# Attention and two mixture stages on one core: first loads on two queues, products with v one batch later, v loaded a pair later

## The chip, the cores and the metric

The kernel runs on one core of one Trainium2 chip. The metric is the device time of one execution in microseconds (us), the median of three runs.

## The reference

Three stages follow one another: windowed attention with sink tokens, a dense layer pair with a softmax-gated unit and a layer norm, and a sum over eight experts. The change touches the first stage alone.

```
batch, n_heads, seq, head_dim = (2, 8, 768, 64);  n_sink, window = (4, 128)
scores = scale * np.matmul(q, k.transpose(0, 1, 3, 2))
keep = (pos[None, :] < n_sink) | ((rel >= 0) & (rel < window))     # rel = query - key
scores = np.where(keep, scores, -1000000000.0)
a = np.exp(scores - np.max(scores, axis=-1, keepdims=True))
a = a / (np.sum(a, axis=-1, keepdims=True) + 1e-09)
x = np.matmul(a, v)                              # (2, 8, 768, 64), then 1536 tokens x 512
h = x @ w_in;  solu = h * softmax(h);  x = layernorm(solu) * g_ln @ w_out
out = sum over e of P[:, e:e+1] * (np.maximum(x @ w1[e], 0.0) @ w2[e])   # P: 8 Sinkhorn rounds
```

## The kernel before

**Tiling.** The 16 heads of attention are worked as 8 pairs (p = 0 to 7); the two heads h of a pair lie on partitions 0 to 63 and 64 to 127 of `q_sb` and `k_sb`. Each head has six query tiles of 128 rows (t = 0 to 5). A tile needs its own 128 keys, the 128 before them and the four sink keys: 128, 256 and then 260 columns. The buffers `q_sb`, `k_sb`, `v_sb`, `v_sink` and `probs` exist twice, one for even and one for odd pairs.

**What happens to a pair.** Every engine runs a program of its own, in which the work is written out in the order in which it is to run; semaphores tie the programs together.

- TensorE: `scores(p, t)` (line 643) makes the scores of a tile for both heads into four banks in turn. `turn(p, b)` (line 663) transposes the probabilities of batch b (tiles 2b and 2b+1; three or four blocks a head) into one of two banks. `turn_sinks(p)` (line 673) does that for the sink columns of tiles 2 to 5. `pv(p, b)` (line 689) multiplies batch b with v, and `pv_sinks(p)` (line 695) adds the sinks and closes the pair (`x_full`).
- VectorE: `mask_max` (line 1179) reads the scores out of their bank, masks them and finds the maximum; `normalise(p, b)` (lines 1187, 1191, 1194) makes the reciprocals of the sums of batch b and scales one tile; `copy_pT` (line 1200) copies the second head's transposes out, `copy_sinkT` (line 1205) those of the sinks; `rest_x(p)` (line 1210) makes the low part of the pair's result and frees its banks (`x_out`).
- ScalarE: `exp_tile` (line 962), `copy_pT` of the first head (line 969), `scale_probs` (line 977) and `round_x(p)` (line 981), the high part of the result, for which `rest_x` waits.
- GpSimd: constants and masks first (lines 458 to 485), then `normalise(p, b)` for the second head (line 493), and between these the split of one eighth of `w_in` and of `w_out` (a segment each) per pair into a high part (`round_segments`, lines 500 and 503) and a rest (`rest_w_in`, line 509, `rest_w_out`, line 515), all from the one buffer `w_raw`.
- SyncE issues all DMAs: `load_qk` (lines 372 to 379, eight DMAs a pair), `load_v` (lines 383, 384, four DMAs a pair), `load_segments` (lines 389, 390). `load_segments(p)` waits until `rest_w_out(p - 1)` has let go of `w_raw`.

**Order.** TensorE runs `scores` one tile ahead of the rest: for each t it does `scores(p, t + 1)` (after t = 5 `scores(p + 1, 0)`) and then `back(p, t)`, which holds the turns and products. In `back` of the kernel before, `turn(p, 0)` stands at t = 4, `pv(p, 0)` at t = 5, and in the next pair `turn(p, 1)` at t = 0, `pv(p, 1)` at t = 1, `turn_sinks(p)` and `turn(p, 2)` at t = 2, `pv(p, 2)` and `pv_sinks(p)` at t = 3. `pv(p, 0)` writes the banks that `rest_x(p - 1)` has to have read. The ScalarE and VectorE programs have a `back` of the same shape. After pair 7 TensorE goes on with the first product of the dense stage, `h1_half(0, 0)` (lines 717 to 719), and does the last turns and products between the four halves of `h1_half`.

In what follows S1 to S5 and S0 are `scores`, T0 to T2 `turn` and V0 to V2 `pv` of batches 0 to 2, K is `turn_sinks` and VK `pv_sinks`, with the pair in brackets: V0(3) is `pv(3, 0)`.

Of the kernel before, what the change touches and what calls it, by code (L numbers as in the profile page):

```python
# [60 lines left out]
def solu_moe(nc: bass.Bass, n_sink, window, qT, kT, v, w_in, w_out, g_ln, w_gate, w_exp, out):  # L61
# [5 lines left out]
    with ExitStack() as ctx:  # L67
# [144 lines left out]

        qk_loaded = [sem(f"qk_loaded{h}") for h in range(2)]
# [152 lines left out]

        @block.sync
        def _(sp):
# [27 lines left out]
            sp.wait_ge(consts, 4)  # L396
# [59 lines left out]
        def _(pool):  # L456

            pool.memset(ident[:, :], 0.0).then_inc(consts, 1)
            pool.memset(ones[:, :], 1.0).then_inc(consts, 1)
            pool.memset(v_sink[:, :], 0.0).then_inc(consts, 1)  # L460
            pool.memset(wg[:, :, :].bitcast(F32), 0.0).then_inc(consts, 1)
            pool.wait_ge(consts, 4)
            pool.affine_select(out=ident[:, :], in_=ident[:, :], compare_op=ALU.not_equal, fill=1.0,
                               base=0, pattern=[[-1, P]], channel_multiplier=1).then_inc(consts, 1)
            pool.memset(mask0[:, :], 0.0)
            pool.memset(mask1[:, :], 0.0)
            pool.memset(mask2[:, :], 0.0).then_inc(masks, 1)
            pool.wait_ge(masks, 1)
# [16 lines left out]
            pool.memset(mask1[:, 0:NS], 0.0).then_inc(masks, 1)  # L485

# [144 lines left out]
        def _(pe):  # L631
            def scores(p, t):

                if t == 0:
                    pe.wait_ge(qk_loaded[p % 2], 128 * (p // 2 + 1))
# [62 lines left out]
            def back(p, t):  # L698
# [40 lines left out]

            pe.wait_ge(consts, 5)  # L740
            scores(0, 0)
# [14 lines left out]
            back(PAIRS, 3)  # L756

# [200 lines left out]
        def _(act):  # L958
            def exp_tile(p, k):
# [23 lines left out]
            def back(p, t):  # L983

                if t == 0 and p > 0:
# [10 lines left out]
            for p in range(PAIRS):  # L996
                for t in range(QT):
                    if t == 4 and p > 0:
                        round_x(p - 1)
# [3 lines left out]
                if p == 0:  # L1003
                    act.wait_ge(small_loaded, 32)
                    act.activation(wg[:, :, WG_AT:WG_AT + EXPERTS], wg_raw[:, :, :], ACT.Copy).then_inc(wg_ready, 1)
# [165 lines left out]
        def _(dve):  # L1171
# [41 lines left out]
            def back(p, t):  # L1213

                if t == 0 and p > 0:
                    normalise(p - 1, 2)
                    copy_pT(p - 1, 1, 1)
                if t == 2:
                    normalise(p, 0)
                    if p > 0:  # L1220
                        copy_sinkT(p - 1)
                        copy_pT(p - 1, 2, 1)
                if t == 4:
                    normalise(p, 1)
                    if p > 0:
                        rest_x(p - 1)
# [14 lines left out]
            normalise(PAIRS - 1, 2)  # L1241
            copy_pT(PAIRS - 1, 1, 1)
# [266 lines left out]
```

## Time and profile before

| | us |
|---|---|
| median of 3 runs | 1272.03 |
| lowest, highest | 1271.93, 1273.18 |
| time of the profiled execution | 1272.06 |
| its span | 1270.3 |
| TensorE (PE) busy in the span | 1243.7 (98%) |
| VectorE, ScalarE, GpSimd busy | 690.2, 363.2, 525.5 |
| first matmul starts | 8.74 |
| first product of the dense stage starts | 110.59 |

The profiled execution is 0.03 us above the median, and 1.76 us of it lie outside its span. Times in rows are us from the span's start; the number behind the count in square brackets is the time for which the engine sat idle before the row, with what ended it. In the rows PE is TensorE, PEld its weight loads, DVE VectorE, ACT ScalarE, POOL GpSimd and SPq the DMA issues of SyncE. The attention stage is the stretch from 0 to 110.59 us; the other 1160 us are TensorE work almost without a gap.

### The profile page before, as it was taken

The page shows a single profiled execution, that of the slowest core. Times are in us where ns is not written, and L with a number is a line of the kernel's source. Part 1 is how long each engine was busy: PE and PEld are TensorE (multiplying, and loading weights), DVE is VectorE, ACT ScalarE, POOL GpSimd, SP SyncE. Part 2 cuts the span into 40 slices and gives each one's busy share as a digit, 9 for nine tenths or more (in the row PEclk, how much of TensorE's full clock was granted, in tenths as well). Part 3 has the DMA queues.
Part 4 walks back from the last instruction along what each step waited for, and adds up shares of the span by engine and source line. Part 5 has one row for each costly group of instructions (what it writes and reads, how often), then busy time and mean ns, then how long its engine had stood idle before and what let it go on. Part 6 is the DMA issues. An engine that isn't in the chain of part 4 may idle for free.

```text
span 1270.3 us, 18733 instructions
## 1 busy us (share of the span) xinstructions
PE 1243.7 (98%) x6462; PEld 1099.9 (87%) x6462; DVE 690.2 (54%) x1347; ACT 363.2 (29%) x823; POOL 525.5 (41%) x576
## 2 busy tenths in 40 slices
PE   5889999999999999999999999999999999999998
PEld 3556899998998999999999999999999999999997
DVE  4886645335665555555555555555555555555554
ACT  4775544332224222222222222222222222222221
POOL 4553222643444444444444444444444444444441
PEclk8999999999999999999999999999999999999999
DMA  6561000011111111111111111111111111111102
GB/s 160 156 158 47 1 1 1 15 36 34 34 34 34 34 34 34 34 33 33 33 33 33 33 33 33 33 33 33 33 36 35 40 38 33 33 33 34 34 17 100
DMA packets 62606, 53.16 MB, mean 42 GB/s; under 512 B 9824, under 2 KB 49760, under 8 KB 62560
## 3 DMA queue, kind: packets, MB, share of 16 engines
q1 hardware_dynamic: 62560, 52.57, 14.1%
q8 instruction: 27, 0.44, 0.1%
q14 instruction: 19, 0.16, 0.0%
HBM read 49.40 MB, written 3.15 MB: 41 GB/s over the span
## 4 chain that ended last, share of the span: by engine, by line
PE 93%; DVE 2%; ACT 2%; SPq 1%; POOL 1%; issue 1%; DMA 0%; DVEq 0%; ACTq 0%
PE ps L717 29%; PE ps L719 29%; PE ps L718 29%; PE ps L689 1%; PE ps L663 1%; PE ps L767 1%; PE ps L643 1%; DVE pT L1200 1%; PE ps L695 1%; POOL probs L493 1%; ACT probs L962 1%; PE ps L900 1%; ACT acc L1127 1%; ACT xw L981 0%; DVE xw L1210 0%
## 5 line engine op out<-in xcount | busy, mean ns | idle before, releaser
L1433 DVE SCALAR_TENSOR_TENSOR acc<-ps,gate_now,acc 128x512 f32<-128x512 f32 x336 | 252.3, 751 | 166.1 <-PE ps L719 162.0
L717 PE MATMUL ps<-ring 128*128 128x512 f32 x768 | 300.6, 391 | 0.0
L718 PE MATMUL ps<-ring 128*128 128x512 f32 x768 | 299.7, 390 | 0.0
L719 PE MATMUL ps<-ring 128*128 128x512 f32 x768 | 299.2, 390 | 0.0
L1109 ACT ACTIVATE sums<-ps 128x384 f32<-128x384 f32 x192 | 94.4, 492 | 596.9 <-PE ps L719 596.9
L1409 DVE TENSOR_TENSOR sums<-ps,sums 128x384 f32<-128x384 f32 x192 | 106.9, 557 | 158.3 <-ACT sums L1109 107.1
L719 PEld LDWEIGHTS ps<-ring 128*128 128x128 f32 x768 | 144.3, 188 | 30.8
L717 PEld LDWEIGHTS ps<-ring 128*128 128x128 f32 x768 | 144.2, 188 | 27.9 <-DVE acc L1429 0.4
L718 PEld LDWEIGHTS ps<-ring 128*128 128x128 f32 x768 | 144.2, 188 | 25.8
L571 POOL TENSOR_TENSOR w_raw<-w_raw 128x256 f32<-128x256 f32 x32 | 23.7, 742 | 322.7 <-PE ps L719 322.7
L717 PE MATMUL ps<-xw,ring 128*128 128x384 f32 x448 | 152.4, 340 | 0.3 <-ACT sums L1109 0.2
L1415 DVE SCALAR_TENSOR_TENSOR ring<-sums,ring 128x384 fp32r<-128x384 f32 x192 | 112.0, 584 | 73.0 <-ACT ring L1120 73.0
L719 PE MATMUL ps<-xw,ring 128*128 128x384 f32 x448 | 151.0, 337 | 0.0
L718 PE MATMUL ps<-xw,ring 128*128 128x384 f32 x448 | 150.9, 337 | 0.0
L717 PE MATMUL ps<-xw,w_b 128*128 128x384 f32 x448 | 150.5, 336 | 0.0
L719 PE MATMUL ps<-xw,w_b 128*128 128x384 f32 x448 | 150.4, 336 | 0.0
L718 PE MATMUL ps<-xw,w_b 128*128 128x384 f32 x448 | 150.0, 335 | 0.0
L600 POOL TENSOR_SCALAR ring<-w_in 128x1024 fp32r<-128x1024 f32 x32 | 33.8, 1056 | 232.7 <-PE ps L719 178.0
L1120 ACT ACTIVATE ring<-sums 128x384 fp32r<-128x384 f32 x192 | 100.2, 522 | 86.5 <-DVE sums L1409 86.5
L717 PEld LDWEIGHTS ps<-xw,ring 128*128 128x128 f32 x448 | 84.1, 188 | 2.6 <-ACT sums L1109 0.5
L718 PEld LDWEIGHTS ps<-xw,w_b 128*128 128x128 f32 x448 | 84.3, 188 | 2.0
L717 PEld LDWEIGHTS ps<-xw,w_b 128*128 128x128 f32 x448 | 84.1, 188 | 1.9
(140 smaller groups left out, 1758.6 us busy)
## 6 DMA issues: line engine op xcount, KB each, us to landing
w_in<-w_exp SPq DMA_DIRECT2D x64, 256.0 KB, 3.2
w_raw<-w_exp SPq DMA_DIRECT2D x64, 128.0 KB, 2.5
w_raw<-w_exp SPq DMA_DIRECT2D x32, 256.0 KB, 3.2
q_sb<-qT SPq DMA_DIRECT2D x16, 192.0 KB, 3.6
k_sb<-kT SPq DMA_DIRECT2D x16, 192.0 KB, 3.9
v_sb<-v SPq DMA_DIRECT2D x16, 192.0 KB
out<-acc SPq DMA_DIRECT2D x12, 256.0 KB, 2.0
k_sb<-kT SPq DMA_DIRECT2D x16, 128.0 KB, 3.6
```

Source lines behind the costliest of these rows:

```text
L493: last = pool.tensor_tensor(a, a, a_stat[:, A_INV, k:k + 1].to_broadcast([P, width(t)]), ALU.mult)
L571: pool.tensor_tensor(raw(4), raw(0), raw(3), ALU.add).then_inc(w1_sums, 1)
L600: pool.tensor_scalar(w2c(0, 0, 2 * BANK), w2_raw(0, 2 * BANK), 1.0, 0.0, ALU.mult, ALU.add).then_inc(w2_hi, 1)
L643: pe.matmul(bank(k % S_BANKS)[:, 0:w], q_sb[rows_h, p % 2, t * P:(t + 1) * P], k_sb[rows_h, p % 2, k_at(t), at:at + w], start=True, stop=T ...
L717: pe.matmul(o, ws[0], xs[0], start=first, stop=False, skip_group_check=True)
L718: pe.matmul(o, ws[0], xs[1], start=False, stop=False, skip_group_check=True)
L719: return pe.matmul(o, ws[1], xs[0], start=False, stop=last, skip_group_check=True)
L1109: act.activation(part_sum(m, s), a_bank(s), ACT.Copy).then_inc(part_copied, 1)
L1120: act.activation(h_at(0, i, b * BLK, BLK), a_bank(s) if m == C12 else c_sum(m), ACT.Relu).then_inc(h_hi_out, 1)
L1409: dve.tensor_tensor(c_sum(m), at, part_sum(part, s), ALU.add).then_inc(c_summed, 1)
L1415: dve.scalar_tensor_tensor(out=h_at(1, i, b * BLK, BLK), in0=a_bank(s) if m == C12 else c_sum(m), scalar=0.0, in1=h_at(0, i, b * BLK, BLK) ...
L1433: dve.scalar_tensor_tensor(out=acc[:, T, :], in0=y_bank(u, T), scalar=gate_now[:, T:T + 1], in1=acc[:, T, :], op0=ALU.mult, op1=ALU.add).t ...
```

## The change

1. **First loads.** The q and k of pair 0 are loaded by `load_first_qk`, for head 0 from SyncE's queue and for head 1 from ScalarE's, six DMAs each in three groups: what tiles 0 and 1 need, what tile 2 needs, the rest. TensorE waits for the group that a tile needs. The masks are made before the identity and the other constants, `scores(0, 0)` runs before the wait for these, and `round_segments(0)` and `rest_w_in(0)` move on GpSimd behind `normalise(0, 1)`.
2. **Products one batch later.** `pv(p, 0)` moves from t = 5 to t = 1 of the next pair, `pv(p, 1)` from t = 1 to t = 3, `pv(p, 2)` and `pv_sinks(p)` from t = 3 to t = 5; `round_x` and `rest_x` move from t = 4 to t = 0 of the pair after.
3. **Sinks.** `turn_sinks` and `copy_sinkT` move from t = 2 to t = 1.
4. **v.** In the loop over pairs SyncE loads v of pair p - 1 instead of pair p behind the segments of pair p; v of the last pair comes after the loop.

```diff
+            queue.dma_start(q_sb[rows_h, 0, 0:front], q_h[:, 0:front]).then_inc(qk_first, 16)
+            queue.dma_start(k_sb[rows_h, 0, 0, at:at + n], k_h[:, 0:n]).then_inc(qk_first, 16)
...
-            for h in range(2):
-                load_qk(0, h)
+            load_first_qk(sp, 0)
...
-                if p >= 2:
-                    sp.wait_ge(x_full, p - 1)
+                if p >= 3:
+                    sp.wait_ge(x_full, p - 2)
                     for h in range(2):
-                        load_v(p, h)
+                        load_v(p - 1, h)
+            sp.wait_ge(x_full, PAIRS - 2)
+            for h in range(2):
+                load_v(PAIRS - 1, h)
...
-            round_segments(0)
             for p in range(PAIRS):
                 normalise(p, 0)
-                rest_w_in(p)
+                if p > 0:
+                    rest_w_in(p)
                 normalise(p, 1)
+                if p == 0:
+                    round_segments(0)
+                    rest_w_in(0)
                 rest_w_out(p)
...
                 if t == 1 and p > 0:
-                    pv(p - 1, 1)
+                    turn_sinks(p - 1)
+                    pv(p - 1, 0)
                 if t == 2 and p > 0:
-                    turn_sinks(p - 1)
                     turn(p - 1, 2)
                 if t == 3 and p > 0:
+                    pv(p - 1, 1)
+                if t == 4:
+                    turn(p, 0)
+                if t == 5 and p > 0:
                     pv(p - 1, 2)
                     pv_sinks(p - 1)
-                if t == 4:
-                    turn(p, 0)
-                if t == 5:
-                    pv(p, 0)
...
-            pe.wait_ge(consts, 5)
             scores(0, 0)
+            pe.wait_ge(consts, 5)
...
+            load_first_qk(act, 1)
```

TensorE, from `scores(2, 2)` to `scores(2, 4)` before (L643 scores, L689 `pv(1, 1)`, L673 `turn_sinks(1)`, L663 `turn(1, 2)`):

```order
L643 MATMUL ps<-k_sb,q_sb 128x260 [waits scores_read] x2
L689 MATMUL ps<-pT,v_sb 64x128 [waits pT_dve,pT_act]
L689 MATMUL ps<-pT,v_sb 64x128
L689 MATMUL ps<-pT,v_sb 64x256 x2
L643 MATMUL ps<-k_sb,q_sb 128x260 [waits scores_read] x2
L673 MATMUL ps<-ident,probs 8x128 [waits probs_scaled,pT_act,probs_ready1,probs_ready0]
L673 MATMUL ps<-ident,probs 8x128 x3
L663 MATMUL ps<-ident,probs 128x128 [waits pT_dve,probs_scaled,probs_ready0]
L663 MATMUL ps<-ident,probs 128x128 x3
L663 MATMUL ps<-ident,probs 128x128 [waits pT_dve,probs_ready1]
L663 MATMUL ps<-ident,probs 128x128 x3
L643 MATMUL ps<-k_sb,q_sb 128x260 [waits scores_read] x2
```

The same stretch now (L672 scores, L702 `turn_sinks(1)`, L718 `pv(1, 0)`, L692 `turn(1, 2)`):

```order
L672 MATMUL ps<-k_sb,q_sb 128x260 [waits scores_read] x2
L702 MATMUL ps<-ident,probs 8x128 [waits probs_scaled,pT_act,probs_ready1,probs_ready0]
L702 MATMUL ps<-ident,probs 8x128 x3
L718 MATMUL ps<-pT,v_sb 64x256 [waits v_loaded1,x_out,pT_dve,pT_act]
L718 MATMUL ps<-pT,v_sb 64x256
L718 MATMUL ps<-pT,v_sb 64x128 x2
L672 MATMUL ps<-k_sb,q_sb 128x260 [waits scores_read] x2
L692 MATMUL ps<-ident,probs 128x128 [waits pT_dve,probs_scaled,probs_ready0]
L692 MATMUL ps<-ident,probs 128x128 x3
L692 MATMUL ps<-ident,probs 128x128 [waits pT_dve,probs_ready1]
L692 MATMUL ps<-ident,probs 128x128 x3
L672 MATMUL ps<-k_sb,q_sb 128x260 [waits scores_read] x2
```

Between `scores(2, 2)` and `scores(2, 3)` the products of batch 1 have given way to the turn of the sinks and the products of batch 0, which bring the waits for v (`v_loaded`) and for the banks (`x_out`) with them; the copies for which `turn(1, 2)` and `pv(1, 1)` wait lie a step further back.

SyncE before, the end of `load_qk(2, 1)` and then the segments and v of pair 2:

```order
L376 DMA k_sb<-kT 64x2x256
L379 DMA k_sb<-kT 64x5x4
L389 DMA w_raw<-w_in 128x512 [waits out_done,in_done]
L390 DMA w_raw<-w_out 128x512
L383 DMA v_sb<-v 128x384 [waits x_full]
L384 DMA v_sink<-v 4x64
L383 DMA v_sb<-v 128x384
L384 DMA v_sink<-v 4x64
```

Now, the end of `load_qk(3, 1)` and then the segments of pair 3 and the v of pair 2:

```order
L394 DMA k_sb<-kT 64x2x256
L397 DMA k_sb<-kT 64x5x4
L407 DMA w_raw<-w_in 128x512 [waits out_done,in_done]
L408 DMA w_raw<-w_out 128x512
L401 DMA v_sb<-v 128x384 [waits x_full]
L402 DMA v_sink<-v 4x64
L401 DMA v_sb<-v 128x384
L402 DMA v_sink<-v 4x64
```

What follows the segments is the v of the pair before; its first use, `pv(2, 0)`, stands at t = 1 of pair 3.

GpSimd before, the start of pair 0 (L500 and L503 round the segments, L493 normalises, L509 and L515 are the rests):

```order
L500 TENSOR_SCALAR xw<-w_raw 128x512 [waits win_loaded]
L503 TENSOR_SCALAR w_end<-w_raw 128x512 [waits wout_loaded]
L493 TENSOR_TENSOR probs<-probs,a_stat 128x128 [waits norm_link]
L493 TENSOR_TENSOR probs<-probs,a_stat 128x256
L509 TENSOR_TENSOR xw<-w_raw,xw 128x512 [waits in_hi]
L493 TENSOR_TENSOR probs<-probs,a_stat 128x260 [waits norm_link]
L493 TENSOR_TENSOR probs<-probs,a_stat 128x260
L515 TENSOR_TENSOR w_end<-w_raw,w_end 128x512 [waits out_hi]
L493 TENSOR_TENSOR probs<-probs,a_stat 128x260 [waits norm_link]
L493 TENSOR_TENSOR probs<-probs,a_stat 128x260
```

Now (L520 and L523, L513, L529 and L535):

```order
L513 TENSOR_TENSOR probs<-probs,a_stat 128x128 [waits norm_link]
L513 TENSOR_TENSOR probs<-probs,a_stat 128x256
L513 TENSOR_TENSOR probs<-probs,a_stat 128x260 [waits norm_link]
L513 TENSOR_TENSOR probs<-probs,a_stat 128x260
L520 TENSOR_SCALAR xw<-w_raw 128x512 [waits win_loaded]
L523 TENSOR_SCALAR w_end<-w_raw 128x512 [waits wout_loaded]
L529 TENSOR_TENSOR xw<-w_raw,xw 128x512 [waits in_hi]
L535 TENSOR_TENSOR w_end<-w_raw,w_end 128x512 [waits out_hi]
L513 TENSOR_TENSOR probs<-probs,a_stat 128x260 [waits norm_link]
L513 TENSOR_TENSOR probs<-probs,a_stat 128x260
```

Four segment operations in a row stand now between the second and the third `normalise` of pair 0.

## Rows read from the trace of the kernel before

**Rows 1.** The page's fourth part: the chain that ended last, by engine.

```profile
PE 93%; DVE 2%; ACT 2%; SPq 1%; POOL 1%; issue 1%; DMA 0%; DVEq 0%; ACTq 0%
```

**Rows 2.** Waits from 35 to 97 us: engine, tile, line, releaser; total us, times, longest.

```profile
PE ps L689 <- DVE pT L1200: 4.5, 14, 0.5
...
PE ps L663 <- POOL probs L493: 2.1, 5, 0.4
```

**Rows 3.** TensorE in order of time: start, us, line, operation, count, idle before.

```profile
8.74 5.67 PE L643 MATMUL ps<-k_sb,q_sb 64*128 64x128 f32 x24 [8.74 <-DMA k_sb<-kT]
14.34 0.55 PE L663 MATMUL ps<-ident,probs 128*128 128x128 f32 x3
18.27 0.90 PE L663 MATMUL ps<-ident,probs 128*128 128x128 f32 x3 [3.38 <-POOL probs L493]
...
19.87 1.55 PE L689 MATMUL ps<-pT,v_sb 128*64 128x256 f32 x8
...
34.38 0.87 PE L689 MATMUL ps<-pT,v_sb 128*64 128x256 f32 x8 [0.53 <-DVE pT L1200]
```

**Rows 4.** First 35 us, SyncE's DMA issues and GpSimd's work, in order of time.

```profile
0.73 0.58 SPq L372 DMA_DIRECT2D q_sb<-qT  x1
...
1.37 0.58 SPq L374 DMA_DIRECT2D k_sb<-kT  x1
...
5.69 0.10 POOL L485 MEMSET mask<- 128x4 f32 x1
...
12.95 0.33 SPq L389 DMA_DIRECT2D w_raw<-w_in  x1
...
15.98 0.62 POOL L500 TENSOR_SCALAR xw<-w_raw 128x512 fp32r<-128x512 f32 x1 [10.18 <-DMA w_raw<-w_in]
...
18.17 1.27 POOL L509 TENSOR_TENSOR xw<-w_raw,xw 128x512 fp32r<-128x512 f32 x1
...
22.66 1.25 POOL L493 TENSOR_TENSOR probs<-probs,a_stat 128x260 f32<-128x260 f32 x2 [0.84 <-DVE a_stat L1191]
```

**Rows 5.** The tile k_sb, first 30 us: time from issue to landing.

```profile
DMA to landing us min/median/max: 3.3/3.7/4.2
```

**Rows 6.** One-us stretches: busy us by engine, granted clock, DMA share, GB/s.

```profile
2.00:3.00 1.00, 0.00 (x0) 0.00 (x0) 0.00 (x0) 0.01 (x1) 0.75 (x5) 1.00 0.78 215
...
17.00:18.00 1.00, 0.00 (x0) 0.00 (x0) 0.00 (x0) 0.00 (x0) 1.00 (x3) 0.62 0.66 241
...
24.00:25.00 1.00, 0.98 (x7) 0.37 (x5) 0.62 (x2) 0.65 (x2) 0.59 (x1) 0.96 0.99 376
```

**Rows 7.** TensorE in order of time, around the last pair and the stage behind it.

```profile
97.22 0.87 PE L689 MATMUL ps<-pT,v_sb 128*64 128x256 f32 x8 [0.54 <-DVE pT L1200]
98.02 0.70 PE L643 MATMUL ps<-k_sb,q_sb 64*128 64x256 f32 x4
98.66 1.09 PE L663 MATMUL ps<-ident,probs 128*128 128x128 f32 x8
...
105.03 1.30 PE L689 MATMUL ps<-pT,v_sb 128*64 128x256 f32 x12 [0.24 <-DVE pT L1200]
106.26 1.12 PE L695 MATMUL ps<-sinkT,v_sink 8*128 8x512 f32 x2
...
110.59 0.50 PE L717 MATMUL ps<-xw 128*128 128x512 f32 x1
```

**Rows 8.** A ten-us stretch in the repeating part: busy us of each engine.

```profile
60.00:70.00 10.00, 9.10 (x68) 5.32 (x64) 8.24 (x34) 7.11 (x25) 5.56 (x9) 1.00 0.76 200
```

**Rows 9.** VectorE in order of time: the copy behind the last batch's transposes.

```profile
104.19 0.69 DVE L1200 COPY pT<-ps 128x512 f32<-128x512 f32 x1 [0.81 <-PE ps L663]
```

**Rows 10.** SyncE's DMA issues in order of time: last segments, last v, first expert weights.

```profile
96.85 0.33 SPq L389 DMA_DIRECT2D w_raw<-w_in  x1
...
109.42 0.38 SPq L426 DMA_DIRECT2D w_raw<-w_exp  x1
```

**Rows 11.** A quarter-us stretch: the last bytes of the last v.

```profile
101.50:101.75 0.25, 0.25 (x3) 0.22 (x4) 0.25 (x3) 0.25 (x1) 0.02 (x1) 1.00 0.06 15
```

More of the change, by code:

```diff
@@ L364, in solu_moe, with load_first_qk @@
         block = ctx.enter_context(nc.Block())
+        def load_first_qk(queue, h):
+            rows_h = slice(64 * h, 64 * h + 64)
+            q_h, k_h = qT[0, h][0:DH], kT[0, h][0:DH]
+            n, at, front = 2 * P, h * NS, 3 * P
+            queue.dma_start(q_sb[rows_h, 0, 0:front], q_h[:, 0:front]).then_inc(qk_first, 16)
+            queue.dma_start(k_sb[rows_h, 0, 0, at:at + n], k_h[:, 0:n]).then_inc(qk_first, 16)
+            queue.dma_start(k_sb[rows_h, 0, QT // 2:QT - 1, at:at + n],
+                            k_h[:, P:SEQ - P].rearrange("d (a n) -> d a n", n=n)).then_inc(qk_second, 16)
+            sinks_at = (1 - h) * n
+            queue.dma_start(k_sb[rows_h, 0, :, sinks_at:sinks_at + NS],
+                            k_h[:, 0:NS].unsqueeze(1).to_broadcast([DH, QT - 1, NS])).then_inc(qk_second, 16)
+            queue.dma_start(q_sb[rows_h, 0, front:SEQ], q_h[:, front:SEQ]).then_inc(qk_third, 16)
+            queue.dma_start(k_sb[rows_h, 0, 1:QT // 2, at:at + n],
+                            k_h[:, n:SEQ].rearrange("d (a n) -> d a n", n=n)).then_inc(qk_third, 16)
         @block.sync
@@ L456, in _ @@
         def _(pool):
[L458 to L464, printed above, removed]
             pool.memset(mask0[:, :], 0.0)
@@ L467, in _ @@
             pool.memset(mask2[:, :], 0.0).then_inc(masks, 1)
+            pool.memset(ident[:, :], 0.0).then_inc(consts, 1)
+            pool.memset(v_sink[:, :], 0.0).then_inc(consts, 1)
             pool.wait_ge(masks, 1)
@@ L485, in _ @@
             pool.memset(mask1[:, 0:NS], 0.0).then_inc(masks, 1)
+            pool.wait_ge(consts, 2)
+            pool.affine_select(out=ident[:, :], in_=ident[:, :], compare_op=ALU.not_equal, fill=1.0,
+                               base=0, pattern=[[-1, P]], channel_multiplier=1).then_inc(consts, 1)
+            pool.memset(ones[:, :], 1.0).then_inc(consts, 1)
+            pool.memset(wg[:, :, :].bitcast(F32), 0.0).then_inc(consts, 1)
             def normalise(p, b):
@@ L632, in scores @@
             def scores(p, t):
-                if t == 0:
-                    pe.wait_ge(qk_loaded[p % 2], 128 * (p // 2 + 1))
+                if p == 0 and t == 0:
+                    pe.wait_ge(qk_first, 64)
+                if p == 0 and t == 2:
+                    pe.wait_ge(qk_second, 64)
+                if p == 0 and t == 3:
+                    pe.wait_ge(qk_third, 64)
+                if p > 0 and t == 0:
+                    pe.wait_ge(qk_loaded[p % 2], 128 * ((p + 1) // 2))
                 for h in range(2):
@@ L738, in h1_half @@
                     last.then_inc(h1_full, 1)
+            scores(0, 0)
             pe.wait_ge(consts, 5)
-            scores(0, 0)
             for p in range(PAIRS):
@@ L756, in _ @@
             back(PAIRS, 3)
+            back(PAIRS, 5)
             def turn_ln(b, f):
@@ L983, in back @@
             def back(p, t):
+                if t == 0 and p > 1:
+                    round_x(p - 2)
                 if t == 0 and p > 0:
@@ L997, in _ @@
                 for t in range(QT):
-                    if t == 4 and p > 0:
-                        round_x(p - 1)
                     for h in range(2):
@@ L1216, in back @@
                     normalise(p - 1, 2)
+                    if p > 1:
+                        rest_x(p - 2)
                     copy_pT(p - 1, 1, 1)
+                if t == 1 and p > 0:
+                    copy_sinkT(p - 1)
                 if t == 2:
@@ L1224, in back @@
                     normalise(p, 1)
-                    if p > 0:
-                        rest_x(p - 1)
                     copy_pT(p, 0, 1)
@@ L1240, in _ @@
                                       wg[:, :, WG_AT:WG_AT + EXPERTS].bitcast(F32), ALU.subtract).then_inc(wg_ready, 1)
-            normalise(PAIRS - 1, 2)
-            copy_pT(PAIRS - 1, 1, 1)
+            back(PAIRS, 0)
             TURNED = {4: (0, 0), 5: (0, 4), 7: (1, 0), 8: (1, 4), 10: (2, 0), 11: (2, 4)}
```

5 lines of the change are left out of this document (3 added, 2 removed).

## The prediction

> **What bounds the kernel now.** I read the page's chain first: 93% of it is TensorE [rows 1], so a microsecond counts only where TensorE stands. Then TensorE in order of time: from 110.59 us on it runs the dense stage and the experts almost without a gap [rows 7], and there the change moves nothing. So I ask one question: when does the first product of the dense stage start, at 110.59 before, and what is added behind it? Ahead of it the rows show two kinds of loss. At the start TensorE waits for the loads until 8.74, and for 3.38 us, until 18.27, for GpSimd, which first rounds segments (their DMA was issued at 12.95 and let GpSimd start at 15.98) [rows 3, 4]. In the repeating part a pair takes 12.57 us (pv(1, 0) starts at 34.38, pv(6, 0) at 97.22 [rows 3, 7]), and TensorE waits in it for copies of VectorE; the waits listed from 35 to 97 us make 4.5 + 2.1 us over five pairs [rows 2]. The second of these is put down to GpSimd; by the order of the code it may be the copy of the sinks.
>
> **What the repeating part could gain.** These 6.6 us are 1.3 a pair: 0.54 at pv(p, 0), 0.24 at pv(p, 2) [rows 7], the rest at pv(p, 1) and in turn(p, 2). The new order puts a whole step between each copy and the instruction that needs it, so all of them can go: 12.57 - 1.3 = 11.2. VectorE is not far behind: 8.24 busy us in ten are 10.4 a pair [rows 8], and it has gaps inside normalise. I keep 11.2 us (10.9 to 11.5) for a pair that nothing else holds.
>
> **What the change adds: a loop through SyncE.** This is the term I trust most. v of pair p is now issued behind the segments of pair p + 1, and these wait for rest_w_out(p), which GpSimd does in the second half of pair p. pv(p, 0) needs that v at t = 1 of pair p + 1. And rest_w_out(p + 1) lies behind normalise(p + 1, 1), that behind scores(p + 1, 3), and that on TensorE behind pv(p, 0). So from one pv(p, 0) to the next runs a closed chain:
> - pv(p, 0) 0.80 (97.22 to 98.02), scores 0.64 (98.02 to 98.66), turn 1.09, and 0.03 until VectorE copies: 2.56 us [rows 7].
> - From that copy (104.19) through the four mask_max, normalise, GpSimd's normalise and rest_w_out to SyncE's next issue (109.42): 5.23 us [rows 9, 10]. The same instructions in the same order stand there after the change.
> - From the segments' issue to the landing of the v behind them: for the last pair 96.85 to 101.5, where the bytes end: 4.7 us [rows 10, 11]. There four DMAs of v follow the segments, as now. TensorE's start after it: 0.1.
>
> The sum is 12.6 us, 1.4 more than the free 11.2. For all TensorE cares, the waits for copies are exchanged for one wait of about 1.4 to 1.7 us ahead of pv(p, 0), and the period stays what it was. Before, the v of a pair was issued a pair earlier, while its use moves back by four steps of six at most, so the trace has no such wait: v of pair 7 has its bytes by 101.7 [rows 11], and no row of pv(p, 0) waits for a DMA. Where is the stall in the queue? Behind it on TensorE stands scores(p + 1, 3), so VectorE and ScalarE wait too; GpSimd's segments and SyncE's next q and k (eight issues of 0.64 us, landing 3.7 us later [rows 4, 5]) may make scores(p + 2, 0) some tenths late, but that wait hides them. The loop closes for v of pairs 2 to 6: v of 0 and 1 are loaded at the start, and v of 7 has the dense stage's first products ahead of it. Bounds of its period: 12.2, if the last v lands with its neighbours 0.4 us before the last bytes, and 13.0, if q and k traffic holds it up.
>
> **The start.** First scores: the second DMA of each queue is issued at 1.37 and the shortest landing is 3.3 us [rows 4, 5], so 4.7 in place of 8.74. The masks, done at 5.8 before [rows 4], come first now, and the wait for the constants costs tile 1 some tenths. Whether ScalarE's issues take SyncE's 0.6 us is in no row; at twice that, ScalarE's first exponential would come at about its old time, and TensorE would still meet the wait that follows. For the 4 us gained here are not kept: turn_sinks(0) needs the third normalise of GpSimd, and ahead of that stand now four segment operations in a row. The w_in segment is issued two DMAs of 0.65 us earlier, at 11.65. By issue alone GpSimd starts on it at 14.7; if the 16 DMA engines, which were at a share of 0.78 even early on [rows 6], are the limit, at 15.6. I take 15.1. Two roundings of 0.62, two rests of 1.27 and the normalise of 1.25 [rows 4] make 5.1: turn_sinks(0) at 20.3. Pair 1's q and k, whose last issue is SyncE's fourteenth (0.73 + 13 x 0.65 = 9.2, landed at 12.9), are then long there. TensorE has finished turn(0, 1) and scores(1, 2) by 17 to 17.5, so it stalls nearly 3 us.
>
> Here the Trainium skill speaks against the two queues: "DMA: Bandwidth & Descriptors", section "Rules for kernel authors", says that spreading DMAs over issuing engines saves only issue time, since all run on the same 16 engines. By that the segments land at the late end, 15.6, and the forecast is 0.5 us later; the share of 0.78 at 215 GB/s agrees that there is only a fifth to win.
>
> The clock: after the idle 3.38 us before 18.27 the granted clock was at half by 18 us and back only just after 24.0, 5.8 us after work resumed [rows 3, 6]. At half clock pv(0, 0) took 1.55 us in place of 0.87 [rows 3, 7], so 44% of such a time is lost. I take the same 5.8 us again, a loss of 2.6 us; if the clock stays up, that is gained. From turn_sinks(0) to the end of pv_sinks(0) TensorE has two products of 0.80, three scores of 0.64, a turn of 1.09 and one of six blocks in place of eight (0.82), pv(0, 2) 1.23 (105.03 to 106.26), pv_sinks 1.05 [rows 7], and for the turn of the sinks and the narrow scores(2, 0), which have no row here, an estimate of 0.45 each, under the 0.64 of wider scores: 8.6 us at full clock, so it ends at 20.3 + 8.6 + 2.6 = 31.5. scores(2, 1), turn(1, 1), scores(2, 2) and the sinks take 2.7: pv(1, 0) at 34.2, 0.2 us ahead of its old time.
>
> **The sum.** pv(2, 0) comes one loop later, 0.25 late since VectorE is still behind rest_x: 47.0. pv(6, 0) four loops of 12.6 later: 97.4. From there to the end of pv_sinks(6) TensorE runs pv 0.80, three scores 1.92, turn(6, 2) 1.09, pv(6, 1) 0.80, turn(7, 0) 0.82, pv(6, 2) 1.23 and pv_sinks 1.05 [rows 7]: 7.7 us, and the dense stage starts at 105.1, against 110.59: 5.5 us earlier. pv(7, 0), 0.80 us, was ahead of that point and now lies behind it; the other turns and products of pair 7 stay between the halves of h1_half, and the wait of the second half of turn(7, 2) for the copy of the sinks stays too, since that copy is still behind the first solu on VectorE. So 5.5 - 0.8 = 4.7 us net: 1272.06 - 4.7 = 1267.4 for the profiled execution, 1267.3 as a median. Its own bounds: each loop 0.4 either way gives 2.0, the clock 2.6 down, the segments 0.5: 1264.0 to 1269.5.
>
> **Rivals.**
> - *v is no bound.* If the four DMAs of v land within 3.3 us of the segments' issue, or stand elsewhere in the queue than I read, the pair runs at 11.2: five times 1.4 us more, 1260.3. For it: the waits removed are real. Against: the last v's bytes end 4.7 us after the issue, with nothing else in flight. 12%.
> - *The loop is longer than the old pair*, at 13.1 or more, because the landing takes 5.2 us beside other traffic: five times 0.5 us lost, 1269.5 to 1272, no change that can be told. 9%.
> - *The clock, the other side.* TensorE now stands still in one piece of 1.7 us a pair, not in four small ones. The old idle pieces of 0.5 us cost no clock, that of 3.38 did [rows 3, 7]; 1.7 lies between. If it drops to half in each pair, the loop's first 2.5 us become 4.6 and the rest of the pair's 10.9 us of work nearly doubles; even if only the first part counts, 2.1 us a pair are 10 us over five pairs: 1277.8. It decides from 1.5 us a pair on, where the 4.7 us are used up and 2.5 more lost. 5%.
>
> **How the numbers follow.** Forecast 72%, the rivals 12, 9 and 5%, and 2% for a clock that never drops at the start together with a quicker loop (1262 to 1264). About 0.2%, 2.5 us, is what a measurement can tell from no change. Faster is the forecast, the first rival and the last case, 0.86; same 0.09; slower 0.05. The range takes the forecast's bounds, a part of the longer loop at one end and goes toward the free pair at the other: 1261.5 to 1270.3.
>
> **What the new profile would show.** Right: first scores at 4.7; turn_sinks(0) at 20.3 behind GpSimd; from pair 3 on one idle stretch of 1.5 to 1.9 us before pv(p, 0), every 12.6 us, with SyncE's v issued 3 to 4.7 us before; no wait at pv(p, 1), pv(p, 2) and the second half of turn(p, 2); the dense stage at 105.1. Wrong: pairs of 11.2 us with no such stretch (the loop does not bind), or a granted clock under 1.00 between 35 and 100 us.

## The result and the profile after

The changed kernel takes 1277.16 us (median of 12 runs, 1272.61 to 1283.58) against 1271.98 for the kernel before on the same chips (12 runs, 1271.28 to 1273.54): a ratio of 1.0035, 95% interval 1.0023 to 1.0047. It is slower by 5.2 us, where 4.7 us of gain were forecast. The profiled execution took 1279.32 us, with a span of 1277.5 and a mean granted clock of 0.991.

| | forecast | measured |
|---|---|---|
| first scores | 4.7 | 4.97 |
| turn_sinks(0) | 20.3 | 20.71 |
| pv(1, 0) | 34.2 | 34.95 |
| period from pv(2, 0) to pv(6, 0) | 12.6 | 13.68, 15.08, 15.73, 14.75 |
| first product of the dense stage | 105.1 | 117.40 (before 110.59) |
| time | 1267.3 | 1277.16 |

TensorE of the changed kernel in order of time, at its start (start us, us, engine, line, operation, count, idle before and releaser), which answers to [rows 3]:

```profile
4.97 2.82 PE L672 MATMUL ps<-k_sb,q_sb 64*128 64x128 f32 x12 [4.97 <-DMA k_sb<-kT]
...
18.14 0.91 PE L672 MATMUL ps<-k_sb,q_sb 64*128 64x260 f32 x4 [2.00 <-DVE a_stat L1212]
20.71 1.01 PE L702 MATMUL ps<-ident,probs 128*8 128x128 f32 x4 [1.67 <-POOL probs L513]
```

GpSimd there, the first segment, which answers to the line of 15.98 in [rows 4]:

```profile
15.27 0.62 POOL L520 TENSOR_SCALAR xw<-w_raw 128x512 fp32r<-128x512 f32 x1 [1.91 <-DMA w_raw<-w_in]
```

The start went nearly as forecast: scores begin 3.8 us earlier and the sinks are turned at 20.71, 0.4 us late. TensorE waits there twice, where one wait of nearly 3 us was forecast: 2.00 us at `scores(1, 2)` and then 1.67 for GpSimd. The first of these is for a bank that `mask_max(1, 0)` has to read, and on VectorE that stands behind the part of `w_gate` (L1273), which waits by way of ScalarE for a load:

```profile
16.57 1.30 DVE L1273 TENSOR_TENSOR wg<-wg_raw,wg 128x32 fp32r<-128x32 f32 x1 [2.21 <-ACT wg L1038]
```

The segments reached GpSimd at 15.27, between the 15.1 taken and the 15.6 that the rule on issuing engines in the Trainium skill ("DMA: Bandwidth & Descriptors", section "Rules for kernel authors") would have given; that rule did not decide anything here.

TensorE from pair 1 to the dense stage, the rows of pv(1, 0) to pv(6, 0) and the first product behind them, which answer to [rows 7]:

```profile
34.95 0.87 PE L718 MATMUL ps<-pT,v_sb 128*64 128x256 f32 x8
...
48.99 0.87 PE L718 MATMUL ps<-pT,v_sb 128*64 128x256 f32 x8 [1.35 <-DMA v_sink<-v]
...
62.67 0.87 PE L718 MATMUL ps<-pT,v_sb 128*64 128x256 f32 x8 [2.35 <-DMA v_sink<-v]
...
77.75 1.55 PE L718 MATMUL ps<-pT,v_sb 128*64 128x256 f32 x8 [2.28 <-DMA v_sink<-v]
...
93.48 0.87 PE L718 MATMUL ps<-pT,v_sb 128*64 128x256 f32 x8 [1.61 <-DMA v_sink<-v]
...
108.23 1.55 PE L718 MATMUL ps<-pT,v_sb 128*64 128x256 f32 x8 [1.95 <-DMA v_sink<-v]
...
117.40 0.50 PE L746 MATMUL ps<-xw 128*128 128x512 f32 x1
```

From pair 2 on, TensorE waits once in each pair for the DMA of v, ahead of pv(p, 0), as the loop of the prediction has it, but at a period of 13.7 to 15.7 us. The waits from 35 to 97 us (columns as in [rows 2]) say the same of the whole stretch; the waits for VectorE's copies, 4.5 us there before, are gone:

```profile
PE ps L718 <- DMA v_sink<-v: 7.6, 4, 2.4
...
PE ps L672 <- DMA k_sb<-kT: 1.3, 1, 1.3
```

The loop's links can be read in the same trace. VectorE's copy behind pv(2, 0), and SyncE's issues of the segments (L407) and of the last v (L402) behind them, which answer to [rows 9, 10]:

```profile
51.57 0.69 DVE L1233 COPY pT<-ps 128x512 f32<-128x512 f32 x1 [1.90 <-PE ps L692]
```

```profile
42.74 0.33 SPq L407 DMA_DIRECT2D w_raw<-w_in  x1
...
56.79 0.33 SPq L407 DMA_DIRECT2D w_raw<-w_in  x1
...
58.87 0.34 SPq L402 DMA_DIRECT2D v_sink<-v  x1
...
71.76 0.34 SPq L407 DMA_DIRECT2D w_raw<-w_in  x1
...
87.62 0.33 SPq L407 DMA_DIRECT2D w_raw<-w_in  x1
...
102.67 0.33 SPq L407 DMA_DIRECT2D w_raw<-w_in  x1
```

From pv(2, 0) at 48.99 to the copy 2.58 us (forecast 2.56), from the copy to the segments' issue 5.22 (5.23), and from there to pv(3, 0) at 62.67 5.88 (4.8 with TensorE's start). The first two terms were right to 0.02 us; the third is 1.1 us too short, and in each of the five loops it is 0.8 to 1.5 us too short: 6.25, 5.88, 5.99, 5.86, 5.56.

The second loss is in the clock. One-us stretches (columns as in [rows 6]), behind the wait of 2.35 us:

```profile
64.00:65.00 1.00, 1.00 (x6) 0.47 (x3) 0.00 (x0) 0.00 (x0) 0.63 (x1) 0.50 0.93 185
...
67.00:68.00 1.00, 1.00 (x12) 0.42 (x8) 1.00 (x6) 0.39 (x1) 0.00 (x0) 0.99 0.03 0
```

The granted clock falls to 0.50, the 1.2 GHz level, from about 63.6 to 67, and again from 77.3 to 84, 94.3 to 97.7 and 108 to 111.4. The part of the loop from pv(p, 0) to the segments' issue, 7.80 us at full clock (48.99 to 56.79), then takes 9.09 (62.67 to 71.76), 9.87 and 9.19.

**Where the 12.3 us between 105.1 and 117.40 are:** pv(1, 0) 0.75 late; the landing 5.5 over five loops (1.45, 1.08, 1.19, 1.06, 0.76); the clock 4.75 in three loops (1.29, 2.07, 1.39), less 0.2 for a copy that was taken as late and wasn't; and 1.5 behind pv(6, 0), where 9.17 us (108.23 to 117.40) stand against 7.7, again at half clock. Behind the dense stage's start little moved: span less start is 1160.1 us, 1159.7 before, so pv(7, 0), which now lies there, cost 0.4 us where 0.8 were taken.

The clock's part differs from run to run, and most of the scatter goes with it: 11 us, where the kernel before scatters over 2.3. The four quickest runs (1272.61 to 1273.42) have a mean clock of 0.996 or 0.997, as the runs of before have; the slowest, 1283.58, has 0.989. So with the clock of before the change costs about 1 us, and most of the rest of the median goes with the clock. The match is not exact: one run at 0.996 took 1276.50 us and another at 0.996 took 1273.20.

### The profile page after: what moved, and what is told of

The parts are those of the page before. It is cut to its first block, busy times and chain, and to the rows that moved or that the text cites. A ratio compares the mean times of both kernels' runs of the same rounds, so it can differ in the third digit from the quotient of the medians.

```text
span 1277.5 us, 18739 instructions
## 1 busy us (share of the span) xinstructions
PE 1251.3 (98%) x6462; PEld 1103.2 (86%) x6462; DVE 691.2 (54%) x1347; ACT 363.2 (28%) x823; POOL 525.9 (41%) x576
## 4 chain that ended last, share of the span: by engine, by line
PE 93%; DMA 2%; SPq 2%; ACT 1%; DVE 1%; POOL 1%; issue 1%; DVEq 0%; ACTq 0%
PE ps L746 29%; PE ps L747 29%; PE ps L748 29%; DMA v_sink<-v 1%; PE ps L718 1%; PE ps L692 1%; PE ps L672 1%; PE ps L797 1%; PE ps L930 1%; ACT acc L1160 1%; PE ps L724 0%; POOL probs L513 0%; SPq L401 0%; POOL w_end L535 0%; DMA k_sb<-kT 0%
## 5 line engine op out<-in xcount | busy, mean ns | idle before, releaser
L1142 ACT ACTIVATE sums<-ps 128x384 f32<-128x384 f32 x192 | 94.3, 492 | 597.8 <-PE ps L748 597.8
```

The source lines that it names most:

```text
L1142: act.activation(part_sum(m, s), a_bank(s), ACT.Copy).then_inc(part_copied, 1)
```

## The experiments

### v early again, in the changed kernel

```diff
-                if p >= 3:
-                    sp.wait_ge(x_full, p - 2)
+                if p >= 2:
+                    sp.wait_ge(x_full, p - 1)
                     for h in range(2):
-                        load_v(p - 1, h)
+                        load_v(p, h)
...
```

> The changed kernel, but v of pair p is issued again behind the segments of pair p (after x_full of pair p - 2). Theory (late v closes the loop, 7.8 us of engine work and 5.9 us of landing, and the stall it makes costs clock on top): the wait before pv(p, 0) is gone, the granted clock is 1.00 from 30 us on, a pair takes 11.2 us, the dense stage starts at about 98.5 and the time is 1260 to 1262 us. Rival (moving the products and rest_x back is what spoils the pair, by VectorE or by the clock): the pair stays at 12.6 us or more and the time above 1270.

Measured: 1267.94 us (1265.50 to 1274.66, 7 runs), ratio 0.9964 [0.9949, 0.9978]. The waits for v are gone, and the change becomes a gain, so v as the change loads it is what made it a loss. But more than half of the gain of the free pair is missing: 1267.94 us is no more than the new start alone brings (the next experiment). The profile names another wait. TensorE in order of time:

```profile
66.49 0.49 PE L669 MATMUL ps<-k_sb,q_sb 64*128 64x128 f32 x4 [1.58 <-DMA k_sb<-kT]
...
94.98 0.80 PE L669 MATMUL ps<-k_sb,q_sb 64*128 64x128 f32 x4 [2.66 <-DMA k_sb<-kT]
```

All five scores(p + 1, 0) wait for k, 0.28 to 2.66 us. The prediction had said that q and k may come some tenths late and that the wait for v hides it; with v early it is the next bound. The granted clock fell here too, from about 67 to 74 and from 95 to 104, so these are stalls before other instructions than pv(p, 0).

### The new start alone, in the kernel before

Part 1 of the change, applied to the kernel before:

```diff
-            for h in range(2):
-                load_qk(0, h)
+            load_first_qk(sp, 0)
...
-            round_segments(0)
             for p in range(PAIRS):
                 normalise(p, 0)
...
+            load_first_qk(act, 1)
```

> The kernel before with the new start alone (two queues, three groups, constants and segments moved); products, sinks and v as before. Theory: the start brings the third normalise of GpSimd and with it turn_sinks(0) from 26.7 to about 20.7 us, of which 1 to 3 us go in a spell at half clock; pairs stay at 12.57 us: 1267 to 1269 us. Rival (the start gives nothing, since TensorE waits for segments, pair 1's loads and w_gate in its place): 1270.5 or more.

Measured: 1268.13 us (1267.51 to 1270.55, 8 runs), ratio 0.9971 [0.9960, 0.9982], as expected. In its trace (TensorE in order of time) pv(1, 0) starts 4.42 us earlier than the 34.38 of [rows 3], and the dense stage 4.41 us earlier than 110.59:

```profile
29.96 0.87 PE L715 MATMUL ps<-pT,v_sb 128*64 128x256 f32 x8 [0.54 <-DVE pT L1229]
...
106.18 0.50 PE L743 MATMUL ps<-xw 128*128 128x512 f32 x1
```

The pairs keep their 12.57 us. The start alone is worth about all that I had forecast for the whole change.

### The later products alone, v early

Parts 2 and 3 of the change, applied to the kernel before; loads at the start and v stay as they were:

```diff
-                    pv(p - 1, 1)
+                    turn_sinks(p - 1)
+                    pv(p - 1, 0)
...
-                if t == 5:
-                    pv(p, 0)
```

> The kernel before with its old start and old v loads, but with products a batch later and the sinks a step sooner. Theory: the pair takes 11.2 us, no stall before pv(p, 0); turn_sinks(0) at about 24 us; 1260.5 to 1264 us. Rival (the products' new place is no gain by itself): 1270 to 1274.

Measured: 1270.53 us (1269.79 to 1279.08, 10 runs), ratio 0.9996 [0.9980, 1.0012]: nothing of the 8 to 11 us expected. The waits of TensorE from 35 to 97 us and of SyncE from 0 to 120 us:

```profile
PE ps L643 <- DMA k_sb<-kT: 5.8, 5, 1.7
```

```profile
SPq L383 <- PE ps L695: 4.6, 6, 1.4
```

TensorE, and SyncE, over one pair:

```profile
69.46 0.49 PE L643 MATMUL ps<-k_sb,q_sb 64*128 64x128 f32 x4 [0.92 <-DMA k_sb<-kT]
...
71.11 1.12 PE L695 MATMUL ps<-sinkT,v_sink 8*128 8x512 f32 x2
...
82.07 0.49 PE L643 MATMUL ps<-k_sb,q_sb 64*128 64x128 f32 x4 [1.29 <-DMA k_sb<-kT]
```

```profile
72.27 0.33 SPq L383 DMA_DIRECT2D v_sb<-v  x1
...
73.78 0.50 SPq L372 DMA_DIRECT2D q_sb<-qT  x1
```

The 6.6 us of waits for copies [rows 2] have become 5.8 us of waits for k, and the pair takes 12.4. This is a second loop, over one pair. The narrow scores at 69.46 wait for k; behind them on TensorE stand the last products and pv_sinks (L695), which close a pair (`x_full`); SyncE has waited for that before it issues v (72.27), and the next q and k stand behind v (73.78), eight issues and a landing ahead of the next narrow scores (82.07). The links are 2.81, 1.51 and 8.29 us, 12.61 in all. It is the wait for `x_full` that binds in this trace, not the segments, which SyncE had issued at 70.82. Even with v early the free pair of 11.2 us cannot be had with SyncE's order.

### The later products with late v

The same, with part 4 added:

```diff
...
-                        load_v(p, h)
+                        load_v(p - 1, h)
...
```

> As the run before, but v as in the changed kernel (of pair p - 1 behind the segments of pair p); only the start is the old one. Theory (late v alone makes the loss): a wait of 1.5 to 2.4 us before pv(p, 0) of pairs 2 to 6, pairs of 13.7 us at full clock and up to 15.7 with a spell at half clock, 1274 to 1282 us and scattered by several us. Rival (the new start brings the clock spells): pairs of 13.7 us throughout, clock 1.00 from 35 us on, 1272 to 1274.

Measured: 1278.33 us (1277.78 to 1280.66, 4 runs), ratio 1.0050 [1.0034, 1.0067], 7.8 us above the kernel with v early, and inside the theory's 1274 to 1282. Its profiled execution has full clock in all its pairs up to the last, and so gives the length of the loop without the clock. TensorE, pv(4, 0) to pv(6, 0):

```profile
78.21 0.87 PE L692 MATMUL ps<-pT,v_sb 128*64 128x256 f32 x8 [2.13 <-DMA v_sink<-v]
...
91.64 0.87 PE L692 MATMUL ps<-pT,v_sb 128*64 128x256 f32 x8 [2.10 <-DMA v_sink<-v]
...
105.22 1.55 PE L692 MATMUL ps<-pT,v_sb 128*64 128x256 f32 x8 [2.23 <-DMA v_sink<-v]
```

The periods are 13.22 to 13.59 us from pv(2, 0) on (51.40, 64.62, 78.21, 91.64, 105.22). So the loop alone is 0.6 to 1.0 us a pair longer than the old pair, and waits of 1.5 to 2.1 us did not bring the clock down here, while one of 2.23 did. The full clock in the pairs is what the rival had said, which blamed the new start for the spells at half clock. The old start does not keep them away: in the kernel just before, with v early, the slowest run took 1279.08 us at a mean clock of 0.989. Whether the new start makes them more frequent is not separated here.

### Is it the q and k behind v that hold v up?

SyncE waits until v has landed before it issues the next q and k:

```diff
                         load_v(p - 1, h)
+                    sp.wait_ge(v_loaded[(p - 1) % 2], 64 * ((p - 1) // 2 + 1))
```

> The changed kernel, but SyncE waits until v has landed before it issues the next q and k, so that nothing follows v in the queue. The disputed size is the time from the segments' issue to pv(p, 0), 5.6 to 6.3 us in the changed kernel against my 4.8. Theory A (what follows in the queue slows it): 5.0 us or less. Theory B (a DMA's completion comes about a microsecond behind its last bytes): still 5.4 or more. Either way q and k come later, so scores of t = 0 wait 2 to 4 us a pair and the time is 1280 to 1300.

Measured: 1278.12 us, a single run. SyncE in order of time:

```profile
56.16 0.33 SPq L407 DMA_DIRECT2D w_raw<-w_in  x1
...
58.23 0.34 SPq L402 DMA_DIRECT2D v_sink<-v  x1
61.01 0.49 SPq L390 DMA_DIRECT2D q_sb<-qT  x1
```

With no q or k behind them the four DMAs of v release SyncE 4.85 us after the segments' issue here; the other four pairs have 5.42, 5.25, 5.87 and 4.78, of which one issue of v that took 1.07 us in place of 0.43 is 0.64 in the first and one of 1.82 is 1.39 in the fourth. TensorE starts 0.2 us after: from issue to pv(p, 0) 5.64, 5.47 and 6.09 us where it waited for v. By the numbers put down beforehand this is the second theory, that the landing is long by itself. Without the stretched issues it is 5.0, 5.5 and 4.7, which leans to the first.

A part of the 1.1 us by which the term was short is a misreading of mine: I took the end of the bytes as the landing. In this trace the last bytes of v move at 47.8, 60.7, 77.5, 93.4 and 107.6 us (read in stretches of 0.1 us), and SyncE is released at 48.16, 61.01, 77.90, 93.87 and 108.07, so the release comes 0.3 to 0.5 us behind the last bytes. The rest of the 1.1 us is not divided by these runs. Traffic of q and k is one candidate: from the last issue of v to TensorE's start it is 3.5 to 3.9 us in the changed kernel, with q and k behind, and 2.6 to 3.4 here. Against it as the only cause, the kernel with the old start has the same q and k behind v and takes 5.36 to 5.79 us for the whole term, and the kernel with q and k first and v late (below) has none behind v and takes 5.34 to 6.10. One issue of v that took 0.96 us in place of 0.43 is 0.5 us of the 6.25 in the first loop of the changed kernel.

The Trainium skill ("DMA: Bandwidth & Descriptors", section "Anatomy of one DMA — SWDGE (gpsimd) path") gives about 2 us of fixed cost for a DMA issued by GpSimd, most of it the completion behind the last byte. These DMAs are issued by SyncE, and here the measurement differs: 0.3 to 0.5 us behind the last byte.

### q and k first, v early

The changed kernel with v early as in the first experiment, and q and k of pair p + 1 issued ahead of the segments of pair p:

```diff
-                if p >= 2:
-                    sp.wait_ge(scores_full, STEPS * (p - 1))
+                if p + 1 < PAIRS:
+                    sp.wait_ge(scores_full, STEPS * p)
                     for h in range(2):
-                        load_qk(p, h)
+                        load_qk(p + 1, h)
```

> The changed kernel with v loaded as before (of pair p) and with SyncE issuing q and k of pair p + 1 ahead of the segments of pair p, no longer behind the segments and v. Theory (two loops run through SyncE: the late v, and the q and k of a pair, which queue behind the segments and span two pairs: 13.2 us of engine work, 2.5 us of six issues, 5.1 of eight, 3.7 of landing = 24.5, or 12.3 a pair): with both open there is no wait for a DMA after 35 us, a pair takes 11.2 us, the clock stays at 1.00, 1259 to 1262 us. Rival (VectorE or GpSimd holds the lagged order at 12 us or more anyway): no DMA waits, but 1266 or more.

Measured: 1261.84 us (1261.62 to 1262.09, 4 runs), ratio 0.9917 [0.9900, 0.9933], as expected. TensorE at pv(2, 0), pv(6, 0) and the dense stage:

```profile
45.61 0.87 PE L715 MATMUL ps<-pT,v_sb 128*64 128x256 f32 x8
...
92.10 0.87 PE L715 MATMUL ps<-pT,v_sb 128*64 128x256 f32 x8
...
99.83 0.50 PE L743 MATMUL ps<-xw 128*128 128x512 f32 x1
```

No instruction of TensorE waits for a DMA from 35 us on. The pairs take 11.6 us ((92.10 - 45.61) / 4), 0.4 more than expected, and the four times lie within 0.5 us. The mean clock of all four runs rounds to 1.000, but that figure misses a spell at the start: the products at 21.28 took 1.55 us, the time of half clock, in a stretch whose granted clock the profile gives as 1.00. From 24 us to the dense stage the rows show no such spell. The loop over two pairs in the expectation is not the one that bound with products later and v early, but the move of q and k opens both, and with v early the loop of v is open too. The scatter is gone with the stalls.

### q and k first, v late

The changed kernel with only the q and k moved as above, v late as in the change.

> The changed kernel with only q and k of pair p + 1 moved ahead of the segments; v as in the changed kernel. Theory (the v loop is by itself enough): a wait for v of 1 to 2 us before pv(p, 0) of pairs 2 to 6, from the segments' issue to pv(p, 0) 5.0 to 5.6 us since no q and k follow v in the queue, pairs of 12.9 to 13.4 us plus clock spells, no wait for k: 1271 to 1277. Rival (the q and k behind it are what makes v late): waits under 0.5 us, pairs under 12, below 1266.

Measured: 1287.67 us (1286.77 to 1288.56, 4 runs), ratio 1.0117 [1.0100, 1.0134], over 10 us above what the theory gave. TensorE, and SyncE, around pair 3:

```profile
56.63 0.71 PE L672 MATMUL ps<-k_sb,q_sb 64*128 64x260 f32 x4
...
68.40 1.55 PE L718 MATMUL ps<-pT,v_sb 128*64 128x256 f32 x8 [4.44 <-DMA v_sink<-v]
```

```profile
57.41 0.49 SPq L390 DMA_DIRECT2D q_sb<-qT  x1
...
62.76 0.55 SPq L407 DMA_DIRECT2D w_raw<-w_in  x1
```

The new order closes a third loop that I had not seen: q and k wait for the last scores of the pair (56.63, issue at 57.41), their eight issues put the segments at 62.76, v is behind these, and pv(3, 0) at 68.40 is what the scores of the next pair stand behind. From pv(2, 0) at 49.93 it is 7.5 + 5.35 + 5.64 = 18.5 us. The same move of q and k gains 6 us with v early and loses 10 with v late. What counts is not how late a load is issued but whether its issue stands, on its queue, behind one that waits for the load's own user.

### Late v, but ahead of the segments

The changed kernel with the two blocks of SyncE in the other order; v is still that of pair p - 1:

```diff
+                if p >= 3:
+                    sp.wait_ge(x_full, p - 2)
+                    for h in range(2):
+                        load_v(p - 1, h)
                 sp.wait_ge(in_done, p)
                 sp.wait_ge(out_done, p)
                 load_segments(p)
-                if p >= 3:
-                    sp.wait_ge(x_full, p - 2)
-                    for h in range(2):
-                        load_v(p - 1, h)
```

> The changed kernel with one thing moved: SyncE issues v of the pair before (still a pair later than in the kernel before) ahead of the segments instead of behind them. If the loop is closed by v's place behind the segments, whose issue waits for GpSimd, then v is issued right behind the eight q and k loads (near 51 us for pair 3, needed near 60), TensorE waits for v nowhere, and what is left is the second loop, through q and k, as in e1: waits for k of 0.3 to 2.7 us before scores(p+1,0), and 1265 to 1269 us. Rival: v's lateness by a pair is itself the harm, whatever it stands behind: waits for v of 1 us and more stay before pv(2,0) to pv(6,0), and 1273 to 1278 us.

Measured: 1263.92 us (1263.44 to 1265.84, 4 runs), ratio 0.9940 [0.9923, 0.9956], a little under the range expected. This tells the theories apart best: the same four DMAs, the same pair late, 13 us quicker. SyncE, the first v of pair 3 and the segments, and the waits of TensorE for DMAs from 35 to 97 us:

```profile
48.62 0.61 SPq L401 DMA_DIRECT2D v_sb<-v  x1
...
54.40 0.33 SPq L407 DMA_DIRECT2D w_raw<-w_in  x1
```

```profile
PE ps L672 <- DMA k_sb<-kT: 2.1, 3, 1.0
```

v is issued at 48.62, some 10 us ahead of its use, no instruction waits for it, and the waits for k are smaller than with v early: 2.1 us where they were 6.6. Ahead of q and k stand now the segments, no longer v and its wait for `x_full`. The periods alternate (12.07, 11.34, 12.31 and 11.26 us), which fits a loop over two pairs through the segments: 13.59 us from the narrow scores at 52.86 to the segments' issue at 66.45, and 10.06 to the narrow scores at 76.51. The lateness is harmless; the place behind the segments, whose issue waits for GpSimd, was the whole harm.

### Two attempts at the start

The kernel with q and k first and v early, with the third normalisation of pair 0 ahead of the first segments on GpSimd, the work put off spread over pair 1, and the parts of `w_gate` made on ScalarE and VectorE after pair 1 instead of pair 0:

```diff
-                if p == 0:
-                    round_segments(0)
-                    rest_w_in(0)
...
                 normalise(p, 2)
+                if p == 0:
+                    round_segments(0)
+                    rest_w_in(0)
```

> As the run with both loops open, and besides: the third normalise of pair 0 stands ahead of the first segments on GpSimd, the first rests are spread over pair 1, and the parts of w_gate are made after pair 1 instead of pair 0. Theory (at the start turn_sinks(0) waits for the segments, and scores(1, 2) for w_gate): turn_sinks(0) at 16 to 17.5 us instead of 20.5, no idle stretch over 1.5 us from 14 to 30 us, 3 to 5 us off the run it builds on: 1255 to 1258. Rival (segments then hold up a later normalise of pair 1): the 3 to 5 us come back as waits for GpSimd before 45 us.

Measured: 1259.90 us (1258.39 to 1261.50, 4 runs), ratio 0.9898 [0.9881, 0.9914]: the quickest of all, and 2 us short of what was expected. TensorE, the two turns of the sinks:

```profile
17.23 0.60 PE L705 MATMUL ps<-ident,probs 128*8 128x128 f32 x4 [0.44 <-POOL probs L510]
...
31.23 0.60 PE L705 MATMUL ps<-ident,probs 128*8 128x128 f32 x4 [2.91 <-POOL probs L510]
```

The first comes 3.1 us earlier than with the old order (20.34), and the second gives 2.9 back: the third normalisation of pair 1 stands on GpSimd behind the segments of pair 1, for whose DMA GpSimd waited. So in the last run all three normalisations of each pair but the last come ahead of its segments, and v is issued ahead of the segments. Against the changed kernel:

```diff
                 if p > 0:
-                    rest_w_in(p)
+                    rest_w_out(p - 1)
                 normalise(p, 1)
...
                 if p + 1 < PAIRS:
-                    round_segments(p + 1)
+                    normalise(p, 2)
+                round_segments(p)
+                rest_w_in(p)
+                if p + 1 == PAIRS:
+                    normalise(p, 2)
+                    rest_w_out(p)
```

> The kernel of e7 with GpSimd's work on the segments moved once more: in each pair all three normalisations come before the segments of that pair, their second remainder comes in the next pair, and SyncE issues v ahead of the segments, so that v no longer waits for GpSimd. In e7 turn_sinks(1) waited 2.91 us for a normalisation of GpSimd that stood behind the segments of pair 1, and TensorE then ran at half clock from 31.8 to 36. Theory: this wait goes; turn_sinks(0) stays at about 17.2, pv(1,0) falls from 31.75 to 29, the pairs take 11.4 to 11.8 us, the dense stage starts at 96 to 97.5, and the time is 1256 to 1258.5 us. Rival: the last segments now come after the last normalisation but one, so the dense stage waits for them, or the half-clock spell was paid for by waits that now come elsewhere: 1259.5 to 1263 us.

Measured: 1261.65 us (1257.37 to 1262.14, 4 runs), ratio 0.9906 [0.9887, 0.9925]. TensorE at pv(1, 0), pv(6, 0) and the dense stage:

```profile
32.44 0.87 PE L715 MATMUL ps<-pT,v_sb 128*64 128x256 f32 x8
...
88.80 0.87 PE L715 MATMUL ps<-pT,v_sb 128*64 128x256 f32 x8
...
98.51 0.47 PE L743 MATMUL ps<-xw 128*128 128x512 f32 x1 [1.92 <-issue]
```

The pairs take 11.27 us ((88.80 - 32.44) / 5), the free pair of the prediction. But the dense stage now waits 1.92 us, until GpSimd has made the rest of the last segment of `w_in`, which now comes that late:

```profile
97.15 1.27 POOL L526 TENSOR_TENSOR xw<-w_raw,xw 128x512 fp32r<-128x512 f32 x1
```

And turn_sinks(0) comes at 19.50 and pv(1, 0) at 32.44, where 17.2 and 29 were expected; the rows of TensorE from 12.4 to 20 us have the durations of half clock. Both theories were right in a part. Against the kernel with q and k first nothing is gained that the measurement can tell.

## Why the prediction was wrong

**The start** was right: first scores, turn_sinks(0) behind GpSimd, the spell of half clock and pv(1, 0) came within 0.8 us of the forecast, and the start alone measures about 4 us. It missed the wait behind `w_gate`, which cost little, since TensorE would have waited for GpSimd anyway. Two small sums were off: the five operations of GpSimd add up to 5.0 us, not 5.1, and the four waits of a pair in the rows to 1.4, not 1.3.

**The loop through SyncE** was the right mechanism: its path, the place of its wait, the absence of other waits and two of its three terms hold. The failed step is the third term, "from the segments' issue to the landing of the v behind them ... 4.7 us". It was read from the last pair, where nothing else is in flight and where I took the end of the bytes as the landing. With TensorE's start, for which 4.8 us were taken, 5.6 to 6.25 us were measured; it was 5.4 to 5.8 with the old start, and 4.7 to 5.5 with q and k held back and less the stretched part of two issues. The end of the bytes for the landing explains 0.3 to 0.5 us of that, and the cause of the rest stays open. The term enters five times, so 1.1 us of it are 5.5 us, more than the whole forecast gain. The rival "the loop is longer" had named this with 5.2 us and 9%; with a term known from one quiet instance and multiplied by five, it should have had at least the weight of the forecast.

**The clock rival** gave 1277.8 us at 5%, and the median is 1277.16. It named the right mechanism too, though its arithmetic (2.1 us in each of five pairs, nothing for the landing) is not what happened: the clock fell in four of the pairs of the profiled execution, and in the quickest runs, to judge by their mean clock, hardly at all. Its chance was too low because it was weighed apart from the landing. A longer landing also makes the stall longer (1.5 to 1.9 us forecast, 1.4 to 2.35 measured), so the two losses come together; that the longer stalls are what brought the clock down is plausible, but not shown, since stalls of one length went both ways.

**"That wait hides them"**, said of late q and k, was true for the changed kernel and hid what the order could give: with v early the lagged order waits for k, and parts 2 and 3 without the rest gain nothing. So the rival "v is no bound", 1260.3 us, could not come true either with SyncE's order; it took q and k first to reach 1261.84.

**The free pair** of 11.2 us was right: 11.27 where nothing holds it.

## What to carry to other kernels

Before a load is moved back in a queue, follow what the issue ahead of it waits for; if that leads back to the load's own user, the period is the sum of the loop, however early the load would be by the clock of the old trace. A term that closes in every pass must be taken from a pass under the same traffic and up to the semaphore, not to the last byte, since its error is multiplied. And where a change trades many small waits for a long one on TensorE, price the granted clock together with the wait.

## What the runs showed of the hardware

- Waits of TensorE of 1.6 to 2.7 us, in a stretch where it is otherwise busy, can bring the granted clock to 0.50 for 3 to 10 us, and need not: it fell behind waits of 1.58, 1.61, 2.35 and 2.66 us, and stayed up behind 1.51, 1.83, 2.10 and 2.13. What decides between them isn't settled by these runs. The cost can be read all the same: slower runs mostly have the lower mean clock (1272.61 us at 0.997, 1279.32 at 0.991, 1283.58 at 0.989).
- The granted clock of the profile can miss a spell at the start: with q and k first and v early the eight products at 21.28 us took 1.55 us in place of 0.87 at a stated clock of 1.00. The durations of the rows show it.
- ScalarE's DMA issues of q and k took 0.59 to 0.86 us, SyncE's 0.57 to 0.65, so the second queue nearly halves the time of issue.
- A single issue on SyncE's queue can be stretched: one of v that mostly takes 0.43 us took 1.07 and 1.82. It is not a matter of full DMA engines alone: in the changed kernel one of 1.86 us began at 31.86, with the DMA share at 0.00 from 31 to 32 us and at 0.27 in the next.
- For four DMAs of v issued by SyncE, the semaphore released its waiter 0.3 to 0.5 us after the last bytes had moved.
